# Two feed-forward layers streamed beside top-k attention: weights split once, raw scores on row halves, the mask moved to two engines

## The reference, cut to what matters

```python
scores = scale * np.matmul(q, k.transpose(0, 1, 3, 2))
kth = np.partition(scores, -32, axis=-1)[..., -32:-31]
scores = np.where(scores >= kth, scores, -1e9)
attn = np.exp(scores - scores.max(-1, keepdims=True))
attn = attn / (attn.sum(-1, keepdims=True) + 1e-09)
x = (attn @ v) laid out as [2304, 512]
h = x @ w_in1;  x = np.maximum(0.01 * h, h) @ w_out1
h = x @ w_in2
g = np.where(h >= 1, h, np.where(h <= -1, 0.0, (h + 1) ** 2 / 4))
out = g @ w_out2
```

## Time and profile before

| | |
|---|---|
| Time, median of 3 runs | 1364.26 us (1362.8 to 1365.81) |
| Profiled execution: its time / its span | 1363.44 / 1361.6 us |
| Busy, share of the span | PE 89%, PEld 71%, DVE 76%, ACT 53%, POOL 19% |
| Mean granted PE clock | 0.966 of full speed |
| DMA | 60.29 MB read, 9.44 MB written |

### The profile page before, as it was taken

How to read it: one execution, slowest core, us unless ns; L and a number is a source line. 1 busy time by engine, 2 the same in 40 slices (tenths; PEclk the granted TensorE clock), 3 DMA queues, 4 the chain that set the end, 5 groups by cost and what they waited for, 6 DMA issues and landing times.

```text
span 1361.6 us, 18845 instructions
## 1 busy us (share of the span) xinstructions
PE 1207.6 (89%) x6112; PEld 962.7 (71%) x6112; DVE 1036.6 (76%) x2436; ACT 728.2 (53%) x1497; POOL 256.1 (19%) x215
## 2 busy tenths in 40 slices
PE   3455988999989899898888989989999999999999
PEld 2334766677667677576676767767898888888887
DVE  6999999999999999999999999922444343343432
ACT  4555765665676576576576567443443342432432
POOL 3111421431341142142142133021000000000000
PEclk9667999999999999999999999999999999999999
DMA  3621101201111111110120110032310010100000
GB/s 106 263 90 38 53 29 45 80 28 53 62 39 59 37 52 57 52 52 28 44 80 28 53 55 21 1 121 98 111 47 0 1 62 0 62 0 0 31 0 31
DMA packets 29359, 70.40 MB, mean 52 GB/s; under 512 B 2160, under 2 KB 7280, under 8 KB 28784
## 3 DMA queue, kind: packets, MB, share of 16 engines
q1 hardware_dynamic: 25072, 65.02, 14.4%
q10 hardware_dynamic: 4224, 4.72, 1.0%
HBM read 60.29 MB, written 9.44 MB: 51 GB/s over the span
## 4 chain that ended last, share of the span: by engine, by line
DVE 55%; PE 35%; issue 6%; DMA 2%; ACT 1%; DVEq 1%; POOL 0%; ACTq 0%; POOLq 0%
DVE top L865 26%; DVE work L870 16%; DVE probs L882 11%; PE ps_moe L601 7%; PE ps_scores L601 7%; PE ps_av L578 7%; PE ps_t_rem L578 4%; PE ps_t L578 3%; PE ps_moe L522 3%; PE ps_moe L509 2%; DVE row_inv L860 1%; DVE row_eps L854 1%; DVE neg_max L918 0%; DMA layer_out<-y_stage 0%; DVEq L139 0%
## 5 line engine op out<-in xcount | busy, mean ns | idle before, releaser
L865 DVE MAX8 top<-work 128x8 f32<-128x576 f32 x432 | 310.1, 744 | 0.1
L509 PE MATMUL ps_moe<-x_t,w_in 128*128 128x288 f32 x1024 | 261.3, 408 | 25.0 <-ACT part_b L715 24.5
L522 PE MATMUL ps_moe<-gate,w_out 128*128 128x288 f32 x1024 | 256.5, 406 | 0.0
L509 PEld LDWEIGHTS ps_moe<-x_t,w_in 128*128 128x128 f32 x1024 | 190.5, 190 | 80.4 <-ACT part_b L715 32.4
L522 PEld LDWEIGHTS ps_moe<-gate,w_out 128*128 128x128 f32 x1024 | 191.7, 190 | 48.6
L870 DVE MATCH_REPLACE8 work<-top,work 128x576 f32<-128x576 f32 x288 | 212.7, 739 | 0.0
L647 ACT ACTIVATE scores<-ps_scores 128x576 f32<-128x576 f32 x144 | 93.5, 649 | 163.5 <-DVE probs L882 135.3
L475 PE MATMUL ps_t<-ident,probs 128*128 128x128 f32 x576 | 96.3, 293 | 86.8 <-ACT probs L661 86.8
L661 ACT ACTIVATE probs<-probs,row_inv 128x576 f32<-128x576 f32 x144 | 111.5, 774 | 103.4 <-DVE row_inv L860 103.3
L400 POOL TENSOR_TENSOR gate<-part_a,part_b 128x288 f32<-128x288 f32 x128 | 121.8, 964 | 220.2 <-ACT part_b L715 218.7
L475 PEld LDWEIGHTS ps_t<-ident,probs 128*128 128x128 f32 x576 | 70.3, 148 | 127.5 <-ACT probs L661 114.9
(11 more groups left out here) (91 smaller groups left out, 2125.2 us busy)
## 6 DMA issues: line engine op xcount, KB each, us to landing
k_raw<-kd SPq DMA_DIRECT2D x64, 288.0 KB, 2.8
v_sb<-vd SPq DMA_DIRECT2D x16, 640.0 KB, 3.9
q_raw<-qd SPq DMA_DIRECT2D x16, 576.0 KB, 3.9
layer_out<-y_stage ACTq DMA_DIRECT2D x8, 576.0 KB, 4.0
w_in<-w_in SPq DMA_DIRECT2D x1, 4096.0 KB, 13.1
w_out<-w_out SPq DMA_DIRECT2D x1, 4096.0 KB, 24.1
w_stage<-w_in SPq DMA_DIRECT2D x8, 512.0 KB, 3.7
w_stage<-w_out SPq DMA_DIRECT2D x8, 512.0 KB, 3.4
```

The source lines that it names most:

```text
L509: mm = pe.matmul(ps_moe[:, f % 2, 0:NQ], w_in[:, k, f * P:(f + 1) * P], x_t[:, k, :], start=k == 0, stop=k == CK - 1)
L522: mm = pe.matmul(ps_moe[:, j % 2, 0:NQ], w_out[:, f, j * P:(j + 1) * P], gate[:, f, :], start=f == 0, stop=f == CF - 1)
L865: dve.max(top[:, s % P_SLOTS, 8 * r:8 * r + 8], src).then_inc(dve_step, 1)
```

## The change

Everything from the tiling on is rewritten; the program is written out step by step, without loops.

- **Order.** `make_items` walks through batch, group (rows 0 to 255, then 256 to 575), pair of heads and block of rows. An item is a block of 128 rows of both heads of a pair (two tiles), or the 64 remaining rows of both (one tile, "mixed"): 80 items, 144 tiles as before.
- **Feed-forward.** Both layers run for a chunk of tokens as soon as attention has it: chunks of 256, 320, 256, 320, 576 and 576 tokens, the last two in two sub-chunks of 288. A layer is done in two blocks of 8 hidden tiles: 8 hidden units (12 matmuls for each sub-chunk), then 4 output units (24 matmuls); the second block's outputs are added to the first's by DVE. All products are of the split kind, three one-pass matmuls. `make_plan` deals units out: 4300 ns of PE time for each step from the step at which a chunk is ready; what is left goes into the last entry of the plan. That puts chunk 0 into steps 22 to 42, chunk 1 into 43 to 68, chunk 2 into 69 to 90, chunk 3 into 90 to 115, chunk 4 into 116 to 150, and chunk 5 whole into entry 150, behind attention (144 tiles and a lag of 6 steps).
- **Weights.** 64 pieces of 128 x 512 elements are loaded raw (two buffers), rounded by ACT, subtracted by GpSimd (three buffers) and stored to DRAM as high and low, three pieces for each of the steps 0 to 21. Every chunk then streams all 64 pieces (512 KB each) again through a ring of four.
- **Scores.** q and k are used as they are, in float32. The two heads of a pair lie on the two halves of the 128 rows, and each matmul uses one half. PSUM holds 288 keys of both heads; ACT copies after each such pair.
- **Mask.** DVE writes (score < 32nd) * -1e30, GpSimd adds it to the score, and ACT's exponential reads that sum and gives the row sum itself.
- **Activations.** Layer 1: two ACT `Prelu` and one GpSimd subtraction. Layer 2: two ACT `Relu`, DVE min(r,1)*r, GpSimd add, ACT copy, GpSimd subtraction.

```diff
+EXP_LAG = 5
+MASK_LAG = 4
+INV_LAG = 3
+OUT_LAG = 6
+VECTOR_AHEAD = 2
+W_SLOTS = 4
+BANKS = 3
+G_SLOTS = 3
+RAW_SLOTS = 2
+SPLIT_SLOTS = 3
+PREP_PER_STEP = 3
+FILL = 4300.0
...
+def make_plan():
+    ready = [LAST_OF_GROUP[c.last_gp] + OUT_LAG + 1 for c in CHUNKS]
+    plan, todo, credit = [], 0, 0.0
+    for s in range(ATTENTION_STEPS + 1):
+        groups = [[], [], []]
+        now = []
+        credit += FILL
+        while todo < len(UNITS) and ready[UNITS[todo].chunk.n] <= s and (credit >= UNITS[todo].ns / 2 or s == ATTENTION_STEPS):
+            credit -= UNITS[todo].ns
+            now.append(UNITS[todo])
+            todo += 1
...
 # SyncE
+            def load_raw(i):
+                need(sp, prep_low, i - RAW_SLOTS + 1)
+                sp.dma_start(raw[:, i % RAW_SLOTS, :], wd[i, :, :]).then_inc(raw_loaded[i % RAW_SLOTS], 16)
+            def store_split(i):
+                sp.wait_ge(prep_low, i + 1)
+                sp.dma_start(w_dram[i, :, :, :], split[:, i % SPLIT_SLOTS, :, :].bitcast(F32)).then_inc(split_stored[i % SPLIT_SLOTS], 16)
+            def stream(g):
+                if g >= W_SLOTS:
+                    sp.wait_ge(unit_done, LAST_UNIT_OF_PIECE[g - W_SLOTS] + 1)
...
+                sp.dma_start(w_ring[:, g % W_SLOTS, :, :].bitcast(F32), w_dram[g % PIECES, :, :, :]).then_inc(w_loaded[g % W_SLOTS], 16)
+            for i in range(PIECES):
+                store_split(i)
+                if i + RAW_SLOTS < PIECES:
+                    load_raw(i + RAW_SLOTS)
+                if PIECES // 2 <= i < PIECES // 2 + W_SLOTS:
+                    stream(i - PIECES // 2)
+            for g in range(W_SLOTS, PIECES * len(CHUNKS)):
+                stream(g)
...
 # TensorE, one step
+                if it:
+                    score(it, s - it.first)
+                for u in first:
+                    feed(u)
...
+                if done and done.last == s - OUT_LAG:
+                    transpose(done)
+                for u in second:
+                    feed(u)
+                if s - OUT_LAG in LAST_OF_GROUP:
+                    values(LAST_OF_GROUP.index(s - OUT_LAG))
+                for u in third:
+                    feed(u)
...
 # a score pair
+                    pe.matmul(ps_s[:, 0, 0:PART], q[0:D, rows], k[0:D, c0:c1], start=True, stop=True)
+                    pe.matmul(ps_s[:, 1, 0:PART], q[D:P, rows], k[D:P, c0:c1],
+                              start=True, stop=True).then_inc(scores_done, 1)
...
 # ScalarE, one step ("quiet": a step with no units)
+                if it:
+                    copy_scores(it, s - it.first)
...
+                if quiet and done and done.last == s - OUT_LAG:
+                    copy_transposed(done)
+                for i in prep_pieces(s):
+                    high_piece(i)
+                if closed:
+                    exponential(s - EXP_LAG)
+                for u in first:
+                    event(u)
...
+                if closed and closed.last == s - EXP_LAG:
+                    normalise(closed)
...
 # ScalarE, a hidden unit of layer 2
+                need(act, gate_low_done, u.h - G_SLOTS + 1)
+                    act.activation(part_r[:, slot, 0:u.width], bank(u), ACT.Relu, bias=0.5, scale=0.5)
+                    act.activation(part_o[:, slot, 0:u.width], bank(u), ACT.Relu, bias=-0.5,
+                                   scale=0.5).then_inc(read_by_act, 1)
...
 # VectorE, GpSimd: the mask
-                dve.scalar_tensor_tensor(out=probs[:, slot, :], in0=scores[:, s % S_SLOTS, :],
-                                         scalar=top[:, slot, TOP_K - 1:TOP_K], in1=expo[:, s % E_SLOTS, :],
-                                         op0=ALU.is_ge, op1=ALU.mult,
-                                         accum_out=row_sum[:, slot:slot + 1]).then_inc(masked, 1)
+            def find_drop(t):
+                need(dve, exp_done, t - D_SLOTS + 1)
+                dve.tensor_scalar(drop[:, t % D_SLOTS, :], scores[:, it.n % S_SLOTS, t - it.first, :],
+                                  top[:, t % T_SLOTS, TOP_K - 1:TOP_K], DROPPED, ALU.is_lt,
+                                  ALU.mult).then_inc(dropped, 1)
+            def close_sum(it):
+                dve.wait_ge(exp_done, it.last + 1)
...
+                pool.tensor_tensor(slot, scores[:, it.n % S_SLOTS, t - it.first, :], slot, ALU.add).then_inc(masked, 1)
...
 # VectorE beside a unit
+                if u.hidden and u.layer:
+                    dve.wait_ge(read_by_act, u.by_act)
+                    dve.scalar_tensor_tensor(out=r, in0=r, scalar=1.0, in1=r, op0=ALU.min,
+                                             op1=ALU.mult).then_inc(curved, 1)
+                elif u.added:
+                    dve.wait_ge(unit_done, u.n + 1)
+                    dve.tensor_tensor(y_cols(u), bank(u), y_cols(u), ALU.add).then_inc(read_by_dve, 1)
```

More of the change, by code:

```diff
@@ L126, in chunk_span, with tiles, last @@
-def chunk_span(c):
-    return (0, SHORT) if isinstance(c, int) and c == 0 else (c * WIDE - (WIDE - SHORT), WIDE)
-def full_tile(t):
-    return divmod(t - (t > MIXED), FULL)
+VC = 2 * KC * D + 2 * D
+@dataclass
+class Item:
+    n: int
+    b: int
+    group: int
+    pair: int
+    rows: int
+    col: int
+    first: int
+    mixed: bool
+    gp: int
+    @property
+    def tiles(self):
+        return 1 if self.mixed else 2
+    @property
+    def last(self):
+        return self.first + self.tiles - 1
```

1237 lines of the change are left out of this document (540 added, 697 removed).

## The result

The changed kernel takes 1475.48 us (median of 4 runs, 1473.06 to 1478.14) against 1363.65 for the kernel before: a ratio of 1.082, 95% interval 1.079 to 1.085. It is 8% slower; 1348 was predicted, and 1475 lies outside the range.

What follows compares the result with a forecast made beforehand. Before the change, DVE was taken to bound attention and PE the second layer. Steps 0 to 21 (205 us), 22 to 149 (848), behind attention (294) and 1.8 around gave 1349, stated as 1348; range 1268 to 1430.

Steps and rivals of the forecast that it cites:

- TensorE's matmuls, 814 and 280 us: Whole kernel: feed-forward matmuls take 814 us of PE and attention some 280, with a score pair at 0.72.
- VectorE's 6.0 us a step: Steps 22 to 149: DVE needs 5.6 us bare and 6.0 with units, under PE's 6.2; `find_drop` taken at 0.66.
- A step then takes ...: Steps 0 to 21, splitting weights: 5.7 us buffer loop plus ACT's other work per step, 205 us; bounds 127 and 225.
- The floor is PE's 799: Steps 22 to 149: 799 us of PE, plus 39 for joints and 10 for streamed pieces, 848 in all.
- the joints: Steps 22 to 149: waits at block ends and layer 2 starts, twelve to thirteen at 3 us, 39 together.
- The engines are up to a step apart and can even that out: Steps 22 to 149: neighbouring steps balance PE and DVE loads, avoiding the 887 us of each step's maximum.
- Rival (b), lockstep: Steps 22 to 149: no evening-out, each step takes its maximum, 887 + 39; total 1437, chance 0.28.
- Rival (a): Steps 0 to 21: the weight split hides, 127 us there and 1271 in total; chance 0.2.
- (c): Attention scores: the two heads' halves run one after another, 0.97 us a pair, total 1386; chance 0.08.
- (d): Weight streaming: pieces arrive at half the rate and chunks 0 to 3 wait, total 1470; chance 0.02.
- Behind attention, 294: After attention: 261 us of PE, 27 for slower layer-2 hidden units, 6 for start and end; bounds 265 and 315.
- the ring: Layer-2 hidden units behind attention: ACT waits for the gate of three before, 2.0 us against PE's 1.59.

Runs made afterwards that it cites:

- four_pieces: Changed kernel with only 4 of the 64 weight pieces split and stored, all streamed pieces being among those 4: 1366.5 us, ratio 1.004 to the kernel before.
- top16: Changed kernel with VectorE finding only the 16 largest scores, leaving out two of four `max` and two `match_replace`: 1438.5 us.
- one_product: Changed kernel with two of the three split products of every feed-forward unit left out: 1306.2 us.
- held_units: Changed kernel with sums closed a step later, three raw buffers loaded before the store, four gate slots, and VectorE handling units one unit later: 1376.3 us.
- two_products: Changed kernel with one of three split products (low weights times high input) left out of each feed-forward unit: 1365.7 us.
- gate_slots_4: Changed kernel with four slots instead of three for a hidden unit's parts: 1465.3 us.
- three_raw: Changed kernel with three raw weight buffers instead of two and the next load issued ahead of the store: 1443.8 us.
- spread_and_held: held_units with two weight pieces split per step instead of three and SP's queue in due order: 1363.8 us, ratio 1.002 to the kernel before.

## Why the prediction was wrong, point by point

- **TensorE's matmuls, 814 and 280 us**: nearly right. The one-pass matmuls are 1 to 5% slower than the line through the earlier trace rows, some 22 us with the rest of TensorE's busy time in the middle stretch. Score pairs took 0.69 for 0.72, by another overlap than the one I reckoned with.
- **VectorE's 6.0 us a step**: right at 6.0, by luck (a cheaper `find_drop` against the holding by GpSimd).
- **"A step then takes ..."**: failed in size. That the loop of two buffers sets the pace was right, and four_pieces shows it. Steps 7 to 20 wait for one round each, as I had it, but the round took 6.4 for 5.7 us (the landing of a raw load was the term that was too small) and the rest 5.2 for 4.3: 162 us instead of 140. Steps 1 to 5 wait for one and a half rounds, not one, and the first step's third raw load took 7.2 us to land: with the start, steps 0 to 6 took 75 us instead of 60. With one more in the last step, 205 became 243, +38, beyond the bound of 225.
- **"The floor is PE's 799", and 49 above it**: the middle stretch is 943.4 = 799 + 22 (TensorE's other busy time) + 36 (half clock) + 86 (TensorE idle). I allowed 49 of idle time and nothing for the clock. Of the 86, the joints are 49 for my 39 and the streamed pieces 0.2 for my 10. Some 36 are waits for attention's own stages, which stood in no line of my sum. Nor did the 36 of the clock: TensorE comes back at 1.2 GHz from waits like the one of 3.18 us, and I had read the 0.73 in the first row and used it for the first stretch alone.
- **"The engines are up to a step apart and can even that out"**: failed. It is the sentence in which I chose between forecast and rival. The changed kernel stands 37 us above the higher of the two limits that top16 and one_product show, and held_units, which takes no load away, wins 36 by the order on VectorE alone. These 37 are another account of the same excess, not a term beside the 86 and 36 above.
- **Rival (b), lockstep, 926 for steps 22 to 149**: the nearest case, with 943. Its mechanism (each step takes its maximum) is only half of it. By it, top16 and two_products should have fallen under 875 and 810; they stood at 906 and 890.
- **Rival (a)** is excluded by the first feed-forward matmul at 243 us (130 in it), **(c)** by 0.69, **(d)** by 0.2 us of waits for streamed pieces in the middle stretch of the changed kernel.
- **Behind attention, 294**: right at 288.7, loop 2.02 us, and gate_slots_4 confirms the ring.
- **The sum**: 38 + 95 - 5 = 128 too low. The chance of 0.58 for faster came from (a) at 0.2, which the fixed order of ACT spoke against, and from taking a floor of one engine plus a few joints as a schedule, with VectorE at 6.0 beside 6.2.

## What to carry to other kernels

When two engines need nearly the same time per step, a third one's wait on either of them is part of the sum: list, for each engine, what stands directly behind an instruction that may wait, and who waits for that. A producer and its small consumer step (here a reciprocal) should not stand behind work for another stream. A joint that idles TensorE is to be priced with the slower clock behind it. And a preparation that is squeezed ahead of the main loop needs a price of its own, with its loop of buffers and landings: here the 64 pieces (0.75 MB of traffic each) cost 110 us, as much as the whole loss.

## What the runs showed of the hardware

- A curve of VectorE (`scalar_tensor_tensor`, the same SBUF tensor as both inputs) that started 0.04 us behind GpSimd's mask took 1.65 us instead of 0.43; 39 such curves ended 0.28 to 0.35 us behind the GpSimd instruction beside them. `find_drop` (`tensor_scalar`) was held as well, at most 1.62 us instead of 0.51; `max` and `match_replace` never.
- Behind waits of 3.18 and 4.32 us (at 313 and 334 us) TensorE ran at 1.2 GHz for 6.8 us each. In one_product, with a third of the feed-forward matmuls left, the mean granted clock of the middle stretch was 0.81.
- Two float32 score matmuls on the two halves of the rows ran side by side, 0.35 us for 288 columns in each of two passes.
- A store of 512 KB landed in 2.8 us (median) in the changed kernel, with the queues at 234 GB/s, and in 5.1 in three_raw at 272; a window of 50 us reached 325 GB/s (the start of spread_and_held).
